# Moving the gate's square, logits and scale steps in a fused attention, expert and feed-forward kernel

## The reference

```python
def _moe_ref(x, expert_emb, tau, w1, w2):
    xn = x / (norm(x) + 1e-06)
    en = expert_emb / (norm(expert_emb) + 1e-06)
    logits = xn @ en.T / tau
    expert_idx = argmax(logits, axis=1)
    probs = softmax(logits)            # with 1e-09 added to the sum
    gate_w = probs[arange(N), expert_idx]
    for e in range(E):
        mask = expert_idx == e
        h = maximum(x[mask] @ w1[e], 0.0)
        out[mask] = gate_w[mask, None] * (h @ w2[e])
```

## Time and profile before

| | |
|---|---|
| time, median of 3 runs | 1480.91 us (1478.43 to 1480.96) |
| the profiled execution | 1480.91 us, its span 1479.2 us |
| granted TensorE clock, mean | 0.961 |
| TensorE busy | 1370.2 us, 93% of the span |
| VectorE busy | 659.6 us, 45% |
| ScalarE busy | 511.4 us, 35% |
| GpSimd busy | 162.0 us, 11% |
| chain of waits | PE 80%, DVE 6%, issue 4%, ACT 3%, DMA 3% |

### The profile page before, as it was taken

How to read it: one execution, slowest core, us unless ns; L and a number is a source line. 1 busy time by engine, 2 the same in 40 slices (tenths; PEclk the granted TensorE clock), 3 DMA queues, 4 the chain that set the end, 5 groups by cost and what they waited for, 6 DMA issues and landing times.

```text
span 1479.2 us, 22797 instructions
## 1 busy us (share of the span) xinstructions
PE 1370.2 (93%) x6879; PEld 1125.7 (76%) x6880; DVE 659.6 (45%) x1680; ACT 511.4 (35%) x977; POOL 162.0 (11%) x200
## 2 busy tenths in 40 slices
PE   3787677999999999997999999999999999999995
PEld 2555466888888887886888888888888888888884
DVE  2775654466655466466532322423223232322322
ACT  2654423355544355353422222222222222222221
POOL 1121231011111011015000100101001010100101
PEclk8887779999999999998999999999999999999998
DMA  7355135144433144223110010101001010010000
GB/s 217 90 122 93 52 63 189 48 171 170 164 110 115 44 147 152 82 55 145 37 43 1 22 36 0 57 0 55 2 0 57 0 57 0 21 36 0 29 0 29
DMA packets 75490, 100.21 MB, mean 68 GB/s; under 512 B 44312, under 2 KB 44856, under 8 KB 74432
## 3 DMA queue, kind: packets, MB, share of 16 engines
q1 hardware_dynamic: 62784, 69.72, 15.9%
q0 software_dynamic: 7200, 20.08, 4.1%
q10 hardware_dynamic: 5472, 9.96, 1.7%
HBM read 71.24 MB, written 28.66 MB: 68 GB/s over the span
## 4 chain that ended last, share of the span: by engine, by line
PE 80%; DVE 6%; issue 4%; ACT 3%; DMA 3%; SPq 1%; DVEq 1%; another core or an unknown queue 1%; ACTq 0%; POOL 0%; POOLq 0%
PE bank_a L1450 25%; PE bank_n L1469 13%; PE bank_t L1469 12%; PE bank_n L1403 11%; PE bank_a L1372 10%; DMA xg<-x_tok,g_idx 2%; PE bank_t L1383 2%; DVE w_lo L963 1%; PE bank_t L1190 1%; PE bank_n L1354 1%; PE bank_a L1173 1%; PE bank_n L1261 1%; PE bank_n L1231 1%; DVE gc L801 1%
## 5 line engine op out<-in xcount | busy, mean ns | idle before, releaser
L1125 DVE TENSOR_TENSOR sq<-rel 128x512 f32<-128x512 f32 (+1 forms) x144 | 95.5, 663 | 486.3 <-ACT rel L764 486.3
L764 ACT ACTIVATE rel<-bank_a 128x512 f32<-128x512 f32 (+1 forms) x144 | 82.8, 575 | 541.6 <-PE bank_a L1450 541.6
L1450 PE MATMUL bank_a<-y_hi,w_in_hi 128*128 128x512 f32 (+1 forms) x576 | 217.7, 378 | 0.1
L1450 PE MATMUL bank_a<-y_hi,w_in_lo 128*128 128x512 f32 (+1 forms) x576 | 217.3, 377 | 0.0
L1450 PE MATMUL bank_a<-y_lo,w_in_hi 128*128 128x512 f32 (+1 forms) x576 | 217.3, 377 | 0.0
L1403 PE MATMUL bank_n<-w_hi,hid_hi 128*128 128x512 f32 x296 | 117.9, 398 | 9.8 <-DVE hid_lo L979 8.3
L1450 PEld LDWEIGHTS bank_a<-y_hi,w_in_hi 128*128 128x128 f32 x576 | 108.3, 188 | 21.4 <-issue 0.8
L1450 PEld LDWEIGHTS bank_a<-y_lo,w_in_hi 128*128 128x128 f32 x576 | 108.3, 188 | 20.7 <-issue 0.2
L1450 PEld LDWEIGHTS bank_a<-y_hi,w_in_lo 128*128 128x128 f32 x576 | 108.3, 188 | 19.9
L1403 PE MATMUL bank_n<-w_hi,hid_lo 128*128 128x512 f32 x296 | 116.8, 395 | 0.0
L1469 PE MATMUL bank_n<-wo_hi,g_hi 128*128 128x512 f32 x288 | 112.5, 391 | 0.7 <-DVE g_lo L1128 0.7
(11 more groups left out here) (231 smaller groups left out, 2114.0 us busy)
## 6 DMA issues: line engine op xcount, KB each, us to landing
w_raw<-in_moe_w SPq DMA_DIRECT2D x16, 2048.0 KB, 7.7
moe_tok<-yg ACTq DMA_DIRECT2D x38, 256.0 KB
x_tok<-x_rows SPq DMA_DIRECT2D x8, 1088.0 KB, 5.5
x_m<-in_x SPq DMA_DIRECT2D x8, 1024.0 KB
y_rows<-moe_tok SPq DMA_DIRECT2D x8, 1024.0 KB
win_raw<-in_moe_w_in SPq DMA_DIRECT2D x8, 512.0 KB
w_raw<-in_moe_w_out SPq DMA_DIRECT2D x1, 4096.0 KB
slot_tab<-ids,pos POOLq DMA_INDIRECT x40
```

The lines of the kernel that those rows point to most:

```text
L764: nc.scalar.activation(rel[:, k, 0:cols], ps_g[k][:, 0:cols], ACT.Relu).then_inc(rel_ready, 1)
L1125: nc.vector.tensor_tensor(sq[:, 0:cols], rel[:, k, 0:cols], rel[:, k, 0:cols], ALU.mult).then_inc(sq_ready, 1)
L1450: last = nc.tensor.matmul(ps_g[n % 2][:, 0:cols], w[:, wc], a[:, c, 0:cols], start=(c == 0 and w is w_in_hi and a is y_hi), stop=(c == DC ...
```

## The change

Only the order of calls changes, in the prologue and in the loop's body, on ScalarE and VectorE; no instruction is added or taken away, and TensorE, GpSimd and SyncE keep their order.

```diff
             x_hi(0)
             gate_square(0)
+            gate_square(1)
             hidden(0)
             x_hi(1)
             hidden_hi(0)
-            gate_square(1)
             hidden(1)
-            gate_soft(0)
             hidden_hi(1)
+            act.wait_ge(st_stored, 16 * B)
             act.wait_ge(tab_ready, 1)
             next_w1(1)
-            act.wait_ge(st_stored, 16 * B)
+            gate_soft(0)
             result(0)
             store(0)
             x_hi(2)
...
             gate_soft(2)
+            gate_square(3)
             hidden(2)
             x_hi(3)
-            gate_square(3)
             next_w1(2)
             hidden_hi(2)
+            gate_square(4)
             win_hi(0)
             next_w2(1)
-            gate_square(4)
             gate_soft(3)
...
             def tile(g):
                 hidden(g + 1)
                 x_hi(g + 2)
+                next_w1(g + 1)
                 gate_square(g + 3)
-                next_w1(g + 1)
                 result(g)
...
             nc.vector.tensor_copy(tile_tab[:], tab_o[:]).then_inc(tab_ready, 1)
-            gate_scale(0)
             dve.wait_ge(slot_tr, 1)
             nc.vector.tensor_copy(idx_all[:], bank_r[:, E:E + 3 * TQ]).then_inc(idx_ready, 1)
-            gate_final(0)
-            gate_scale(1)
 
 
             hidden_lo(1)
             dve.wait_ge(tab_ready, 1)
             next_w1(1)
+            gate_scale(0)
+            gate_final(0)
             x_lo(2)
             gate_logits(2)
+            gate_scale(1)
             gate_final(1)
             gate_scale(2)
+            gate_logits(3)
             gate_final(2)
             x_lo(3)
-            gate_logits(3)
+            gate_scale(3)
             next_w1(2)
             hidden_lo(2)
+            gate_logits(4)
             win_lo(0)
             next_w2(1)
-            gate_logits(4)
-            gate_scale(3)
             gate_final(3)
...
             def tile(g):
                 x_lo(g + 2)
-                gate_logits(g + 3)
                 gate_scale(g + 2)
                 next_w1(g + 1)
                 hidden_lo(g + 1)
+                gate_logits(g + 3)
                 next_w2(g)
```

## The result

| | before | after |
|---|---|---|
| time, median of 5 runs each on one chip | 1478.43 us (1474.95 to 1480.96) | 1490.87 us (1487.78 to 1493.85) |
| ratio | | 1.0087, 95% interval 1.0061 to 1.0111 |
| the profiled execution | 1480.91 us | 1486.57 us, its span 1484.9 us |

The changed kernel is slower by 0.0087 x 1478.4 = 12.9 us (9.0 to 16.4). So the two spans can't be subtracted; I compare stages.

The account below looks back on a forecast made before the run. TensorE, busy 93% of the span, was taken to bound the kernel. The terms -0.8 - 0.7 + 7.2 + 3.6 + 3.1 + 0.8 = +13.2 us took 1480.91 to 1494.1 us, range 1482 to 1503 us.

Parts of the forecast that it names:

- tile C: Second loop tile after tile A; its gather was to start later yet land 0.5 to 2 us before it is wanted.
- w_lo 0.12 us earlier: VectorE's loop: moving gate_logits from in front of w_lo starts it 0.12 us earlier, seven times, -0.8 us.
- tile A: Loop tile in which the next expert's weights are converted; 13.36 us against an ordinary 12.25, foretold to stay at 13.2.
- The wait of 0.68 us: VectorE's one wait for the gather in a tile A, no longer standing before w_lo: -0.7 us.
- Part 1: VectorE's loop: tile A's gather is issued behind the 2 MB w1 load; TensorE waits 1.2 us, six times, +7.2 us.
- Part 2: ScalarE's loop: the square waits for the late gather and delays the work behind it; 0.6 us six times, +3.6 us.
- tile B: Loop tile following tile A; ScalarE's square and result were to run late there, making TensorE wait 0.6 us.
- Part 4: Last tiles: a gather must wait for hidden_lo and lands late beside the 4 MB w_out load, +0.8 us.
- Part 3: Prologue: gate chains behind hidden_lo(1) delay result(0), x_hi(2), x_lo(2) and the next gathers, +3.1 us.
- Rival 1: Loop gathers share the queues evenly with the load and land in time: +1.6 us, 1482.5 us, chance 0.13.
- Rival 2: Each new wait also takes TensorE's clock to its lower level, adding 9.6 us: 1503.7 us, chance 0.10.
- Rival 3: Tile A on VectorE: next_w1's register loads run ahead of the gate chain, w_lo starts earlier: 1475.5 us, chance 0.11.

Follow-up runs that it names:

- e4: Changed kernel with loop loads of w1 cut to the first of four blocks (0.5 MB instead of 2 MB): ratio 0.9978 to the kernel before.
- e12: Changed kernel with two small DMAs, one after the other, ahead of each loop load of w1 on SyncE: ratio 0.9997 to the kernel before.
- e1: Kernel before with only VectorE's loop move, gate_logits(g + 3) behind hidden_lo(g + 1): ratio 1.0130.
- e7: Changed kernel with TensorE's expert register for up(g + 1) loaded at the tile's start, ahead of turn_hidden: ratio 1.0071 to the kernel before.
- e2: Kernel before with only the changed prologue on VectorE and ScalarE, loop moves left out: ratio 0.9974.
- e5: Changed kernel with one small DMA ahead of each loop load of w1 on SyncE: ratio 1.0145 to the kernel before.
- b_again: Kernel before, unchanged, timed and profiled a second time: ratio 0.9997.
- e6: Kernel before with next_w1's two register loads on VectorE moved to the tile's start, ahead of x_lo(g + 2): ratio 1.0004.
- e3: Kernel before with only ScalarE's loop swap, next_w1(g + 1) ahead of gate_square(g + 3): ratio 0.9993.
- e10: Kernel before with VectorE's loop rotated so that next_w1's two register loads are issued ahead of hidden_lo: ratio 0.9949.
- e8: Kernel before with the prologue's gate_scale(1) on VectorE moved from in front of hidden_lo(1) to behind gate_logits(2): ratio 0.9992.
- e11: Kernel before with the edits of e10 and e8 together: ratio 0.9917.

## Why the prediction was right, and where it wasn't

The forecast was +13.2 us, measured +12.9. The sign was right, and so was the mechanism in the loop: gathers late behind the weight loads. That the sum came within 0.3 us is luck: two errors of opposite sign met, 3.7 us missed in tiles C and 3.1 us put down for the prologue that the runs don't show.

- **w_lo 0.12 us earlier:** right. From one turn of the hidden rows to the next tile A took 304.53 - 291.31 = 13.22 us, 0.14 less. The last change, which no load follows, went from 13.35 to 13.21 us.
- **The wait of 0.68 us**: gone. That interval was 14.19 us in before and is 14.35 in after, like the other five (14.19 to 14.38), which were 13.36 to 13.41.
- **Part 1, the gather behind the load:** right, in mechanism and size. Issue 2.2 us behind the load (2.1 foretold), landing 6.28 us (6.34), extra time before turn_x 2.00 - 0.88 = 1.12 us (1.2) at the first of six tiles. The wait itself was 0.76 to 0.98 us, a little under the "over 1 us" foretold. e4 and e12 show the cause. The 3.51 us taken as undisturbed had a DMA share of 0.73 over its stretch (245.0 to 248.5 us), so it was not quite that; but in e1 three landings at a share of 0.28 to 0.34 took 3.46 to 3.50 us, and the figure holds. In the view by windows (columns as in the earlier trace rows: stretch, length, busy time of the engines, granted clock, DMA share, GB/s) the second row covers most of the time in which the gather was under way (300.20 to 306.48 us), at a DMA share of 0.93 and 368 GB/s; the others are used below:

```profile
227.09:230.50 3.41, 3.41 (x8) 2.73 (x9) 2.50 (x16) 0.40 (x2) 0.95 (x1) 0.50 0.98 383
299.40:305.60 6.20, 6.17 (x32) 4.95 (x30) 3.69 (x19) 0.97 (x2) 0.97 (x1) 1.00 0.93 368
306.53:319.42 12.89, 12.55 (x60) 10.31 (x61) 8.21 (x13) 10.09 (x18) 1.73 (x3) 1.00 0.23 64
```

- **Part 2, ScalarE's pile-up:** right in size, 0.64 us in each tile B (0.6 foretold), but shown as idle time nowhere: TensorE loses the same 0.6 us to its restart behind the stall (one of the 12 exposed register loads in each B, the other in each C), so it comes to turn_x just as x_lo is ready. e7 took the restart away and B stayed; e1 lengthened the pile-up and B grew. Two causes of one size lay over each other. The chain alone gives the 0.64 us (e7); that the restart alone would give it too is inferred from tile C, where it costs 0.6 us.
- **Missed: tile C.** The stall sends a second exposed register load into tile C, 0.6 us six times, 3.7 us in all. e7 shows it. The sum had 10.1 us for the loop (7.2 + 3.6 + 0.8 - 1.5); with tile C it would have been 13.8, and the other terms together came out 0.8 us smaller, which gives the 13.0.
- **Part 4, the tail:** right, 13.13 - 12.25 = 0.88 us (0.8 foretold).
- **Part 3, the prologue:** wrong. Foretold +3.1 us. The timed runs less the loop's difference give -3.8 + 0.4 = -3.4 us in e2, -3.2 + 0.7 = -2.5 in e4, -0.4 - 0.5 = -0.9 in e12, 0 in after, 10.5 - 9.0 = +1.5 in e7 and 21.4 - 17.1 = +4.3 in e5, uncertain by 2 us (e2) to 6 us (e5). From the first up() to the turn of the earlier trace rows six profiles with the old prologue took 51.5 us on average (49.0 to 52.6), six with the new one 51.7 (48.7 to 55.8). The kernel in which nothing but the prologue changed, e2, was faster by 1.9 to 5.7 us; over all six kernels the mean is -0.2 us. So a loss of 3 us doesn't show, and whether the new prologue gains anything stays open. The sign named for this part, that the turn at 248.57 moves, looked fulfilled in the two profiles compared first (48.99 us behind the first up() in before, 52.73 in after), but before's was the shortest of the six old ones; the other five took 51.5 to 52.6 us.

The step that failed is "taking gate_scale(0) and (1) from in front of hidden_lo(1) gains nothing: that one starts at 228.13, when its input is there". It was read from one execution, in which slot_sb landed so late that TensorE waited 2.69 us for it and then ran slowly; both gate chains fitted into that delay. In b_again, the same kernel, TensorE waited 1.6 us less for slot_sb and VectorE's chains held it instead. TensorE's timeline, then the granted clock behind it:

```profile
212.81 0.47 PE L1342 MATMUL bank_r<-ident,slot_sb 96*128 96x96 f32 x3 [1.05 <-DMA slot_sb<-slot_tab]
213.06 2.09 PE L1403 MATMUL bank_l<-w_lo,hid_hi 128*128 128x512 f32 x8
214.99 1.03 PE L1383 MATMUL bank_t<-ident,hid 128*128 128x128 f32 x8
219.91 0.79 PE L1403 MATMUL bank_n<-w_hi,hid_hi 128*128 128x512 f32 x1 [3.89 <-DVE hid_lo L979]
```

```profile
219.91:225.20 5.29, 5.29 (x13) 4.13 (x14) 0.54 (x1) 0.00 (x0) 0.18 (x1) 0.50 0.76 218
```

So the old prologue has two courses, which the wait for slot_sb tells apart in these six profiles. "To the turn" is the time from the slots' transposition (L1342) to the turn of the earlier trace rows; it begins when slot_sb has landed, so the last column adds the wait in front of it.

| kernel, prologue | wait for slot_sb | wait at down(1) | to the turn | with the wait |
|---|---|---|---|---|
| before, old | 2.69 | 0.69 | 25.2 | 27.9 |
| e6, old | 2.14 | 0.98 | 25.7 | 27.9 |
| b_again, old | 1.05 | 3.89 | 30.0 | 31.1 |
| e3, old | 0.68 | 4.23 | 30.4 | 31.1 |
| e1, old | 0.29 | 4.63 | 30.8 | 31.1 |
| e10, old | 0 | 5.06 | 30.0 | 30.0 |
| after, new | 0 | 0.98 | 27.3 | 27.3 |
| e2, new | 0.44 | 0.98 | 27.5 | 27.9 |
| e12, new | 0.32 | 0.97 | 27.0 | 27.4 |
| e7, new | 0 | 0.98 | 27.4 | 27.4 |
| e5, new | 0 | 0.98 | 27.6 | 27.6 |
| e4, new | 0 | 0.98 | 26.2 | 26.2 |
| e8, gate_scale(1) moved | 2.23 | 0.98 | 24.8 | 27.0 |
| e11, gate_scale(1) moved | 0 | 0.97 | 26.3 | 26.3 |

By the last column the two courses are 2 to 3 us apart, and the new prologue takes 2 to 5 us less than the slower one and 0 to 2 us less than the faster. No profile has the new prologue with a late slot_sb, the case for which the forecast was worked out.

In the new prologue down(1) starts on time, but what I had foretold happened as well: result(0) and x_hi(2) are late, and up(2) waits 3.92 us instead of 0.57 and then runs at a granted clock of 0.50 (first of the three windows above). The hold of hidden(0) by gate_square(1) lies ahead of the table's stretch and is not always covered either: TensorE's wait for hid was 0.69 us in all six profiles of the old prologue, and 0.69 (e2), 1.68, 1.86, 2.72, 2.86 (after) and 5.41 us (e5) in those of the new one. The losses were real; the gain I had put at nothing was about as large.

**The rivals.** Rival 1 (gathers in time) is out for the changed kernel, and true of e4 and e12. Rival 2 (the clock) is out for the loop: the granted clock is 1.00 from 306.53 to 319.42 us, behind a wait of 0.96. Behind a longer wait it did come: in e5, behind one of 1.94 us at 349.25, it was 0.51, the lower level of 1.2 GHz, and that interval took 14.39 us instead of 12.89. It was one of six such waits of e5; behind the other five (1.26 to 1.78 us) B kept its 12.89 us, and behind the one of 1.78 us the granted clock was 1.00. The row behind the longest:

```profile
350.19:353.60 3.41, 3.41 (x8) 2.74 (x9) 1.06 (x2) 1.51 (x3) 0.01 (x1) 0.51 0.21 83
```

The Trainium skill ("TensorE: Matmul & The Clock Gate", Part 1: The HAM clock gate) has the clock fall to its lower level when the engine was idle; the rows at 0.50 and 0.51 agree, and the loops of after and e5 show that waits of 0.96 and 1.78 us didn't bring it down. Rival 3 (the register loads run ahead by themselves) is out, the row at 293.34 has them still; but its reckoning, that 1.5 us of loads make the 1.11 us, was right, as e10 shows.

**Open.** How the gather loses 2.7 us beside a load wasn't taken apart: waiting behind the load's packets or slower reads of its indices and rows would look alike here. Nor is it known what lets slot_sb land early or late.

## What to carry to other kernels

Before moving a step later, follow the buffer it frees: here one sum of 0.21 us, moved 11 us down its queue (from 3.0 us ahead of turn_hidden, to 7.8 us behind it), made a gather start 6.6 us later, behind a 2 MB load that follows the same w_lo, and cost 13 us. A cover read from one execution ("it is hidden by that wait") needs a second profile if the cover is a DMA's landing; a term put at nothing may have two values from execution to execution. Small register loads are worth moving to where the engine waits anyway in every tile: that gave 7.5 us (e10), where the same loads put in front of x_lo gave none (e6).

## What the runs showed of the hardware

- A gather of 128 rows took 3.3 to 3.6 us from the start of its issue where no 2 MB load ran beside it for long. It took 6.0 to 6.3 us when issued 2.2 us behind a 2 MB load and 6.6 to 7.3 us when issued 0.3 us ahead of it; with the load 3.0 us behind it (e12), the instruction that waits for it started 3.51 us behind the end of the issue, against 3.21 to 3.27 undisturbed. The Trainium skill ("DMA: Bandwidth & Descriptors", Queues, rings and completion order) has each DMA engine take turns between queues packet by packet; by the traces the small transfer still lost 2.7 us beside the large one.
- One register read from a table in SBUF costs TensorE 0.32 to 0.34 us of idle time and some 0.3 us more until the rhythm is back, only in the tiles behind a stall; two cost VectorE 1.48 us in front of w_lo. In a tile without a stall TensorE's read leaves no idle time between turn_x and up() (332.25 and 332.60 us in after).
- Two delays that end together hide each other: taking one away (e7) left tile B at 12.89 us.
- A wait of TensorE does not always cost clock: behind 0.96 us (after) and 1.78 us (e5) the granted clock was 1.00, behind 1.94 us (e5) 0.51 and behind 3.9 us (b_again, after) 0.50.
